# Value products spread over slots 15 to 20, and the last seven slots in a written order

## What is computed

```python
for t in range(S):
    y[:, :, t] = einsum('bhd,bhde->bhe', r_t, state + outer(u * k_t, v_t))
    state = w_t[:, :, :, None] * state + outer(k_t, v_t)
```

```python
h = gelu(x @ w_in)                       # 1024 wide
u, v = h[..., :512], h[..., 512:]
v_n = (v - mean(v)) / sqrt(var(v) + 1e-6) * g_ln
v_s = einsum('ts,bsd->btd', w_sg, v_n) + b_sg[None, :, None]
x = x + (u * v_s) @ w_out
```

## Time and profile before

| | |
|---|---|
| median of 3 runs | 373.62 us (372.19 to 373.78) |
| the profiled execution, its own time | 377.46 us |
| its span | 375.7 us |
| busy: PE, DVE, ACT, POOL | 95%, 63%, 48%, 20% |
| mean granted clock of PE | 0.973 |
| DMA | 23.73 MB, mean 63 GB/s |

### The profile page before, as it was taken

One profiled execution on the slowest core, in us unless ns is written; L12 is line 12 of the kernel. 1 busy time (PEld: TensorE's weight loads), 2 busy tenths in 40 slices (PEclk: granted clock), 3 DMA queues, 4 the chain that ended last, 5 costly groups with the idle time before them and its releaser, 6 DMA issues.

```text
span 375.7 us, 11261 instructions
## 1 busy us (share of the span) xinstructions
PE 358.4 (95%) x4909; PEld 332.9 (89%) x4909; DVE 236.2 (63%) x399; ACT 180.4 (48%) x310; POOL 74.5 (20%) x113
## 2 busy tenths in 40 slices
PE   8997987988799999999999999999999999999996
PEld 6766776877697788999899999999999999999996
DVE  5898778888773789675453679788953116752111
ACT  4754667776644366621240682378648003754000
POOL 6860210221000000000000026039600001951000
PEclk9999899999856999999999999999999999999999
DMA  8587852334210231300000040150000111000011
GB/s 249 161 214 225 248 145 63 85 59 89 56 35 0 36 96 24 75 2 0 0 2 0 2 167 3 29 202 2 0 2 0 44 42 42 2 0 2 21 58 48
DMA packets 39568, 23.73 MB, mean 63 GB/s; under 512 B 25568, under 2 KB 39008, under 8 KB 39520
## 3 DMA queue, kind: packets, MB, share of 16 engines
q1 hardware_dynamic: 39104, 23.02, 22.1%
q10 hardware_dynamic: 416, 0.00, 0.1%
HBM read 18.29 MB, written 2.36 MB: 55 GB/s over the span
## 4 chain that ended last, share of the span: by engine, by line
PE 93%; issue 4%; ACT 1%; DVE 0%; ACTq 0%
PE ps L1308 22%; PE ps L1309 22%; PE ps L1310 21%; PE ps L1298 11%; PE ps L1222 5%; PE ps L1245 3%; PE ps L1277 2%; PE ps L1256 2%; PE ps L1227 2%; PE ps L1232 1%; PE ps L1218 1%; PE ps L1269 1%; ACT yT L754 1%; ACT uT L780 0%; ACT wT L713 0%
## 5 line engine op out<-in xcount | busy, mean ns | idle before, releaser
L1298 PEld LDWEIGHTS ps<-r,kT 48*64 48x64 f32 x1920 | 35.5, 141 | 15.4 <-issue 13.5
L682 POOL TENSOR_TENSOR sq_f<-sq_f 128x384 f32<-128x384 f32 x32 | 33.8, 1072 | 74.9 <-ACT sq_f L824 74.8
L1298 PE MATMUL ps<-r,kT 48*64 48x32 f32 x1920 | 40.2, 226 | 6.8 <-issue 6.7
L1118 DVE TENSOR_TENSOR ot<-ps,ee 128x384 f32<-128x384 f32 x12 | 6.7, 558 | 54.6 <-PE ps L1310 54.6
L951 DVE TENSOR_TENSOR kT<-kT,wb 112x384 f32<-112x384 f32 x40 | 22.5, 564 | 19.1 <-PE ps L1298 18.6
L1103 DVE TENSOR_TENSOR sq_l<-sq_f,sq_h 128x384 fp32r<-128x384 f32 x32 | 27.6, 864 | 10.4 <-ACT sq_h L829 10.4
L1310 PE MATMUL ps<-xk_h,wk_l 128*128 128x384 f32 x96 | 32.2, 335 | 0.0
L1309 PE MATMUL ps<-xk_l,wk_h 128*128 128x384 f32 x96 | 32.2, 335 | 0.0
L1308 PE MATMUL ps<-xk_h,wk_h 128*128 128x384 f32 x96 | 32.2, 335 | 0.0
L1308 PE MATMUL ps<-wv_h,sq_h 128*128 128x384 f32 x96 | 32.1, 334 | 0.0
L1310 PE MATMUL ps<-wv_h,sq_l 128*128 128x384 f32 x96 | 32.1, 334 | 0.0
(11 more groups left out here) (158 smaller groups left out, 899.3 us busy)
## 6 DMA issues: line engine op xcount, KB each, us to landing
vt<-in_v_dram SPq DMA_DIRECT2D x32, 72.0 KB, 2.8
sgn<-in_moe_w_sg_dram SPq DMA_DIRECT2D x18, 128.0 KB, 2.9
out_dram<-ot SPq DMA_DIRECT2D x12, 192.0 KB, 1.9
raw_w<-in_w_dram SPq DMA_DIRECT2D x7, 288.0 KB, 4.3
raw_k<-in_k_dram SPq DMA_DIRECT2D x7, 288.0 KB, 5.0
raw_r<-in_r_dram SPq DMA_DIRECT2D x7, 288.0 KB, 5.4
xT<-yT SPq DMA_DIRECT2D x24, 72.0 KB, 2.3
win_raw<-in_moe_w_in_dram SPq DMA_DIRECT2D x12, 128.0 KB, 4.3
```

Source lines behind the costliest of these rows:

```text
L682: nc.gpsimd.tensor_tensor(t, t, t, ALU.mult).then_inc(k_sq, 1)
L1298: ins = nc.tensor.matmul(to[CHUNK[g], (x * C + c) * cols:(x * C + c + 1) * cols], kU[lo:hi, s] if l == 0 else kT[q % 4][lo:hi, s], rU[lo:h ...
```

## The change

PE's and ACT's lists for slots 14 to 21 are written out in LAST and ACT_LAST. V products stand one in each slot from 15 to 20; U products stand two in slot 20 and six in slot 21. In slot 15 the sg turn stands ahead of level (6,3). In slots 18 to 21 kt, u, yl and y of pairs 6 and 7 stand ahead of more of the early products. The casts of x for batch 0 go one each into slots 12, 13 and 14 on ACT, each waiting only for the stored rows that it reads; the subtractions x_l all into slot 14 on DVE. Statistics are taken one by one in slots 16 to 19, the last two with the norm at the start of slot 20 (ahead of the chain of pair 7); apply_norm for all six at the start of slot 21. Low parts: win_l for U in slots 17 and 18, wsg_l four in slot 19 and two in slot 21 (behind apply_norm). x_l moves behind gtmp in memory, the sgn ring is turned by two, and the waits follow. The warm-up products of pair 7 go.

```diff
         elif slot % 2 == 0:
-            jobs = [("level", a - 2, 4), ("kt", a - 3)] + EARLY_FIRST.get(slot, [])
+            jobs = [("level", a - 2, 4), ("kt", a - 3)]
...
-            (2, 0): 1, (2, 1): 1, **{(q, 1): 2 for q in range(3, NP)}}
-    GATE = {7: [("sg", 0)], 9: [("sg", 1)], 11: [("sg", 2)], 13: [("sg", 3)], 14: [("sg", 4)], 15: [("sg", 5)]}
-    EARLY_FIRST = {18: [("V", 0, 4)], 20: [("U", 0, 3)]}
-    EARLY_DENSE = {16: [("V", 0, 0), ("V", 0, 1)], 17: [("V", 0, 2), ("V", 0, 3)], 18: [("V", 0, 5)],
-                   19: [("U", 0, 0), ("U", 0, 1), ("U", 0, 2)], 20: [("U", 0, 4), ("U", 0, 5)],
-                   21: [("U", 0, 6), ("U", 0, 7)]}
-    ACT_LAST = {18: [("kt", 6), ("wm", 6), ("V", 0, 4), ("sy", 6), ("V", 0, 5)],
-                19: [("root", 0), ("y", 6), ("U", 0, 0), ("vn", 0), ("U", 0, 1), ("vn", 1), ("U", 0, 2), ("vn", 2)],
-                20: [("kt", 7), ("wm", 7), ("vn", 3), ("U", 0, 3), ("vn", 4), ("sy", 7), ("U", 0, 4), ("vn", 5), ("U", 0, 5)],
-                21: [("y", 7), ("U", 0, 6), ("U", 0, 7), ("high", 21)]}
+            (2, 0): 1, (2, 1): 1, **{(q, 1): 2 for q in range(3, NP - 1)}}
+    LAST = {14: [("level", 5, 4), ("kt", 4), ("level", 6, 2), ("sg", 4), ("level", 7, 0), ("u", 4)],
+            15: [("level", 5, 5), ("sg", 5), ("level", 6, 3), ("yl", 4), ("level", 7, 1), ("V", 0, 0), ("y", 4)],
+            16: [("level", 6, 4), ("kt", 5), ("level", 7, 2), ("V", 0, 1), ("u", 5)],
+            17: [("level", 6, 5), ("level", 7, 3), ("V", 0, 2), ("yl", 5), ("y", 5)],
+            18: [("level", 7, 4), ("kt", 6), ("V", 0, 3), ("u", 6)],
+            19: [("level", 7, 5), ("yl", 6), ("V", 0, 4), ("y", 6)],
+            20: [("V", 0, 5), ("kt", 7), ("U", 0, 0), ("u", 7), ("U", 0, 1)],
+            21: [("yl", 7), ("U", 0, 2), ("y", 7)] + [("U", 0, n) for n in range(3, 2 * FT)]}
+    ACT_LAST = {14: [("kt", 4), ("wm", 4), ("sg", 4), ("high", 14), ("x", 2), ("sy", 4)],
+                15: [("sg", 5), ("high", 15), ("V", 0, 0), ("y", 4)],
...
+                20: [("V", 0, 5), ("kt", 7), ("wm", 7), ("root", 0), ("U", 0, 0), ("sy", 7), ("U", 0, 1)],
+                21: [("U", 0, 2), ("y", 7), ("vn", 0)]
+                    + [job for n in range(1, C) for job in (("U", 0, n + 2), ("vn", n))] + [("high", 21)]}
...
-    LOW_SLOTS = {("inv", 0): 9, ("inv", 1): 11, ("inv", 2): 13, ("inu", 0): 16, ("inu", 1): 17, ("inu", 2): 17,
-                 ("sg", 0): 18, ("sg", 1): 18, ("sg", 2): 19, ("sg", 3): 20, ("sg", 4): 20, ("sg", 5): 21,
+    LOW_SLOTS = {("inv", 0): 9, ("inv", 1): 11, ("inv", 2): 13, ("inu", 0): 17, ("inu", 1): 18, ("inu", 2): 18,
+                 ("sg", 0): 19, ("sg", 1): 19, ("sg", 2): 19, ("sg", 3): 19, ("sg", 4): 21, ("sg", 5): 21,
...
-                act.wait_ge(yt_stored, stored_at(PPB * (b + 1) - 1))
+                act.wait_ge(yt_stored, stored_at(PPB * b + min(((m + 1) * P - 1) // (2 * D), PPB - 1)))
...
-                    dve.wait_ge(turned, turn_at[("sg", C - 1)] + 1)
+                    dve.wait_ge(turned, turn_at[("sg", RING)] + 1)
...
                 if slot == 20:
-                    apply_norm(0, range(3, 5))
+                    norm_stats(0, range(4, C))
+                    norm(0)
+                if slot == 21:
+                    apply_norm(0, range(C))
...
-                        if slot == 16:
-                            low_x(0, {4: 1, 2: 2}[l])
+                        if slot == 14 and l:
+                            low_x(0, {4: 0, 2: 1}[l])
...
-                if slot == 15:
-                    low_x(0, 0)
-                if slot == 17:
-                    norm_stats(0, range(4))
-                if slot == 18:
-                    norm_stats(0, range(4, C))
-                    norm(0)
-                if slot == 19:
-                    apply_norm(0, range(3))
-                if slot == 20:
-                    apply_norm(0, range(5, C))
+                if slot == 14:
+                    low_x(0, 2)
+                if 16 <= slot < 20:
+                    norm_stats(0, range(slot - 16, slot - 15))
```

More of the change, by code:

```diff
@@ L57, in pe_jobs @@
             jobs = FILL[slot]
+        elif slot in LAST:
+            jobs = LAST[slot]
         elif slot % 2 == 0:
-            jobs = [("level", a - 2, 4), ("kt", a - 3)] + EARLY_FIRST.get(slot, [])
+            jobs = [("level", a - 2, 4), ("kt", a - 3)]
             jobs += [("level", a - 1, 2), ("w", a + 1)] + GATE.get(slot, [])
@@ L64, in pe_jobs @@
             jobs += GATE.get(slot, []) + [("y", a - 3)]
-        jobs = [job for job in jobs if 0 <= job[1] < NP]
-        return jobs + EARLY_DENSE.get(slot, [])
+        return [job for job in jobs if 0 <= job[1] < NP]
     def side_jobs(slot):
@@ L83, in act_jobs @@
         jobs = [job for job in jobs if job[0] == "high" or 0 <= job[1] < NP]
-        return jobs + EARLY_DENSE.get(slot, [])
+        return jobs + [("x", 0)] * (slot == 12) + [("x", 1)] * (slot == 13)
     FILL = {0: [("level", 0, 0), ("w", 1)],
@@ L98, in rwkv_gmlp_channel_mix_kernel @@
     WARM = {(0, 2): 2, (0, 3): 1, (0, 4): 1, (0, 5): 1, (1, 0): 1, (1, 1): 1, (1, 2): 1, (1, 3): 1,
-            (2, 0): 1, (2, 1): 1, **{(q, 1): 2 for q in range(3, NP)}}
-    GATE = {7: [("sg", 0)], 9: [("sg", 1)], 11: [("sg", 2)], 13: [("sg", 3)], 14: [("sg", 4)], 15: [("sg", 5)]}
-    EARLY_FIRST = {18: [("V", 0, 4)], 20: [("U", 0, 3)]}
-    EARLY_DENSE = {16: [("V", 0, 0), ("V", 0, 1)], 17: [("V", 0, 2), ("V", 0, 3)], 18: [("V", 0, 5)],
-                   19: [("U", 0, 0), ("U", 0, 1), ("U", 0, 2)], 20: [("U", 0, 4), ("U", 0, 5)],
-                   21: [("U", 0, 6), ("U", 0, 7)]}
-    ACT_LAST = {18: [("kt", 6), ("wm", 6), ("V", 0, 4), ("sy", 6), ("V", 0, 5)],
[3 rows of a table removed]
+            (2, 0): 1, (2, 1): 1, **{(q, 1): 2 for q in range(3, NP - 1)}}
+    GATE = {7: [("sg", 0)], 9: [("sg", 1)], 11: [("sg", 2)], 13: [("sg", 3)]}
+    LAST = {14: [("level", 5, 4), ("kt", 4), ("level", 6, 2), ("sg", 4), ("level", 7, 0), ("u", 4)],
[6 rows of a table added]
+            21: [("yl", 7), ("U", 0, 2), ("y", 7)] + [("U", 0, n) for n in range(3, 2 * FT)]}
+    ACT_LAST = {14: [("kt", 4), ("wm", 4), ("sg", 4), ("high", 14), ("x", 2), ("sy", 4)],
[7 rows of a table added]
+                    + [job for n in range(1, C) for job in (("U", 0, n + 2), ("vn", n))] + [("high", 21)]}
     FIRST_TURNS = [("k", 0), ("r", 0), ("w", 0)]
@@ L288, in rwkv_gmlp_channel_mix_kernel @@
         x_h = up("x_h", [P, MT, S], F32R)
-        x_l = up("x_l", [P, MT, S], F32R)
         bbc = up("bbc", [P, S], F32)
         gtmp = [up(f"gtmp{x}", [P, HF], F32) for x in range(2)]
+        x_l = up("x_l", [P, MT, S], F32R)
         assert low[0] == A_aT
@@ L540, in load_sg @@
                 for j in range(3):
-                    sp.dma_start(sgn[:, t % RING, j * 2 * P:(j + 1) * 2 * P],
+                    sp.dma_start(sgn[:, (t + 2) % RING, j * 2 * P:(j + 1) * 2 * P],
                                  w_sg[t * P:(t + 1) * P, j * 2 * P:(j + 1) * 2 * P]).then_inc(sg_in[t], 16)
@@ L588, in _ @@
                     load_last_of_mlp()
-            sp.wait_ge(turned, turn_at[("r", NP - 1)] + 1)
+            sp.wait_ge(turned, turn_at[("sg", C - 1)] + 1)
             sp.dma_start(bbc[:, :], b_sg.rearrange("(a s) -> a s", a=1).broadcast_to([P, S])).then_inc(bias_in, 16)
@@ L877, in _ @@
                         lay_rows(job[1], job[2])
+                    elif job[0] == "x":
+                        high_x(0, job[1])
                     elif job[0] == "root":
@@ L883, in _ @@
                         copy_turn(job)
-                if slot == 14:
-                    for m in range(MT):
-                        high_x(0, m)
             for m in range(MT):
@@ L1232, in turn_job @@
                         ins = nc.tensor.transpose(dst[:, j // 3, (j % 3) * P:(j % 3 + 1) * P],
-                                                  sgn[:, q % RING, j * P:(j + 1) * P], ident[:, :])
+                                                  sgn[:, (q + 2) % RING, j * P:(j + 1) * P], ident[:, :])
                 ins.then_inc(turned, 1)
@@ L1320, in group_job @@
                 elif g < EARLY:
-                    turn_free([job for job in TURNS if turn_banks(job) is turn][-1])
+                    turn_free(("sg", C - 1))
                 if g == EARLY:
```

## The result

The changed kernel takes 378.04 us (377.59 to 381.4, 4 runs) against 373.70 us (372.19 to 374.58, 4 runs): a ratio of 1.014, 95% interval 1.0073 to 1.0207. It is slower. In a later comparison the same pair gave 378.85 against 373.47, 1.0184 (1.0136 to 1.0233). Forecast were 372.4 us and a range of 368.5 to 379: the time lies inside the range, on the other side of no change; slower had been given a chance of 0.30.

A forecast was written before the change was run, and what follows sets the result against it. PE was taken to bound the kernel, with low clock the largest loss ahead of G. Span 375.7 - 3.5 + 2.3 = 374.5, profiled run 376.3, median 372.4 us; range 368.5 to 379.

The forecast's parts named there:

- The steps inside the change: Slots 14 to 21 priced slot by slot at full clock, putting G's start at 150.8 instead of 154.3 us.
- the sum: Slots 14 to 21: priced PE work plus holes of 6.8 us at an unbroken clock, G starting at 150.8.
- 0.8 of code hole: Slot 15, inside level (6,3): late instruction code leaves about 0.8 us of the former 1.46 us hole.
- 0.45 of wait for DVE: Slot 15, after yl and ahead of level (7,1): PE waits 0.45 us for DVE to take level (5,5).
- The assumption that I called decisive: Slots 14 and 15: the clock stays up, as sg turn separates the holes, the longer is halved, dense V follows.
- Rival B: Low clock survives among the spread V products from slot 15 or 16: 375.8, 385 or 397 us; chance 0.18.
- If the first V does: Case where the first V lifts the clock: work from 101.3 to 105.1 takes 3.4 us more, 375.8 us.
- The span becomes 375.7 - 3.5 + 2.3: Whole span: 3.5 us gained ahead of G, 2.3 us lost to the clock, giving 374.5 us.
- about 8.3 went to the clock and small waits: Kernel before, 97.48 to 154.32: of 56.8 us, about 8.3 was clock loss and small waits.
- the 2.3 for the clock: Clock falls at G's start behind the 3.6 us hole: loss between 0 and 4.5 us, taken as 2.3.
- Rival C: Ahead of G: unprofiled runs have shorter code holes, so less to win; 374 to 376 us, chance 0.14.
- rival D: Ahead of G: the spread changes nothing, as PE's work is the same; 373.6 us, chance 0.06.

The follow-up runs named there:

- a_again: The changed kernel unchanged, run again for more runs and a trace: 378.85 us, 1.0184 of the kernel before.
- a_tail: Changed kernel with low parts of w_sg pieces 4 and 5 moved to slot 20 and ACT's vn casts one place earlier in slot 21: 373.17 us, 0.9972.
- a_chain: Changed kernel with low parts of w_sg pieces 2 and 3 moved from slot 19 to slot 20, behind the chain of pair 7: 378.03 us, 1.0086.
- a_slot15: Changed kernel with the first V put ahead of level (7,1) in slot 15: 378.30 us, 1.0088 of the kernel before.
- a_fill: Changed kernel with 16 warm-up products of 512 columns on PE between the last U product and G: 376.71 us, 1.0129.
- a_sg: Changed kernel with only the low parts of w_sg pieces 4 and 5 moved to slot 20, ACT's order kept: 376.26 us, 1.0111.
- a_all: Changed kernel with w_sg pieces 2 to 5 in slot 20, ACT's vn casts two places earlier, V ahead of level (7,1): 371.81 us, 0.9961.
- a_best: a_all with V ahead of yl of pair 6 in slot 19 and U ahead of yl of pair 7 in slot 21: 372.50 us, 0.9916.
- b_look2: The kernel before, unchanged, one more run traced for where its low-clock stretches lie: 381.36 us.
- b_again: The kernel before, unchanged, run and traced again: 373.08 us, 0.9968 of the kernel before.

## Why the prediction was wrong

**The steps inside the change were right.** Forecast and measured in the profile after: hole ahead of yl of pair 6, 0.65 and 0.76; of pair 7, 1.3 and 1.31; ahead of G, 3.6 and 3.72, ended by the subtraction named; a low clock behind G's start, 1.8 and 1.7 us of cost. G was put at 150.8 without low clock ahead of it, 54.4 us behind u, and came at 153.2. The same stretch took 55.55 us in a_again, without low clock: 1.2 us more than the sum, mostly holes (7.65 us against 6.8), among them two waits of 0.23 for ACT's copy of y that the sum doesn't have.

**Slot 15 was half right.** I had 0.8 of code hole and 0.45 of wait for DVE. The code came in time (only 0.11 ahead of yl), so PE was early and waited 1.41 for the same take of level (5,5): the sum is 0.3 off. The assumption that I called decisive, a clock that stays up, failed in this trace:

```profile
102.50:103.00 0.50, 0.50 (x30) 0.89 0.00 0
103.00:103.50 0.50, 0.50 (x2) 0.50 0.00 0
106.00:106.50 0.50, 0.50 (x3) 0.70 0.00 0
```

That is PE's clock by half microseconds in the changed kernel: it fell at 102.9 and was back at 106.3, while the first V ran. It cost 1.7 us. Rival B had "If the first V does", with 3.4 us more; it did, at half that price. In a_again, a_tail, a_chain, a_slot15, a_fill, a_sg, a_all and a_best, all with a V in slot 15, no fall came in slots 15 and 16 at all; a_slot15's came in slot 14. That is one of nine traces with 3.4 us in slots 15 and 16, against two of four with 17. It may be the spreading, but nine and four traces of something that comes and goes don't show it. Nor is the hole shown as the trigger: the same 1.46 us stood ahead of the fall in the forecast's trace and in b_look2, and in b_again no fall came behind it.

**The step that failed is the base of the sum.** "The span becomes 375.7 - 3.5 + 2.3": the 3.5 gained rests on "about 8.3 went to the clock and small waits", and the prediction carried the difference to the median over unchanged. Of those 8.3 us, 5.3 are the low stretch (57.90 against 52.65 us from u to G), which most runs don't have, and the same sum over b_again's rows leaves 3.1 for the rest. So the step counted as gained a low stretch that the typical run doesn't have, and carried that gain over to a median that was free of it. With b_again as the base, the forecast's own 54.4 us from u to G is 1.7 slower than 52.65, and with the 2.3 for the clock 4.0 slower: 377.7 us, where 378.04 was measured. Rival C named this stretch as shorter in the other runs, and priced it at 1.7 us, a third of what the rows show; its heading, shorter code holes, was the wrong cause. The warning was in plain view: the profiled run lay 3.8 us above the median of three runs, and a low-clock stretch was the largest loss in it.

**What the change won and lost ahead of G, at the full clock.** From u to G, b_again's holes add up to 4.2 us: 1.46, 0.32 and 0.56 ended by nothing that the profile shows, 1.26 for the third x_l, and 0.63 in two waits for ACT. In a_again the first kind is down to 0.45 and the wait for x_l is gone; waits for DVE have come in their place, 0.94, 0.76 and 1.32, with 0.46 for ACT: 3.9 in all. As far as the spreading goes that is rival D's case. The tail's 3.72 come on top, and the warm-up products take 0.54 off: 2.9 us, and 55.55 - 52.65 is 2.9. With 1.3 behind G it is 4.2 us slower by these two traces, against 4.3 and 5.4 measured. a_tail takes back 4.9. So the tail is shown as the cause, and the spread V products by themselves moved the typical time by nothing that these runs can tell (a_tail 0.9972, b_again 0.9968).

What the prediction cited from the Trainium skill (TensorE: Matmul & The Clock Gate, "What's actually happening"), that activity releases the throttle, agrees in kind with a_fill, which kept PE active through the tail and its clock at 1.00. It doesn't explain the 17 us at 1.2 GHz in the kernel before, over work that the rows show as busy. "Mostly hidden", said of code supply in the Trainium skill (Runtime: NRT & Kernel Launch, "Instruction fetch mechanics"), fits some stretches (0.11 us in slot 15 of the changed kernel) and not others (1.46 again in slot 15 of b_again).

## What to carry to other kernels

Before a forecast builds on a loss in one trace, ask whether it is in every run: a profiled time well above the median is a warning, and a few more traces of the unchanged kernel price it. Compare traces from one piece of common work to the next, not from the start of the span: ahead of u alone the four traces of the kernel before differ by 3.9 us (96.42 to 100.29). When an order is rewritten, follow the last product's path through every engine to the first consumer of the next stage, and put work that nobody waits for yet (here two subtractions) into the idle time ahead of it. A hole on TensorE is paid twice where the clock falls behind it.

## What the runs showed of the hardware

A hole of 2.09 us ahead of G (a_sg) was followed by 3.4 us at 1.2 GHz, and so was one of 3.72 in each of four traces; 0.53 (a_tail) and 0.25 (a_fill) were not. Elsewhere the hole doesn't decide it: behind 1.46 us in slot 15 the clock fell in two traces of the kernel before and stayed up in a third. Once down in slots 15 and 16 of the kernel before, it took 17 us to come back, through work that the trace shows as busy. It took 3.4 in slot 15 of the changed kernel, with a V product there, and 3.4 in slot 14 of a_slot15, with none. What sets the length is open.

The 17 us at half the clock cost 5.3 to 5.8 us and not 8.5, as waits of PE that stand at the full clock were covered. One kernel's runs differed by 8 us (371.28 to 379.27 in 35 runs of one session), and their mean clock between 0.964 and 0.995.

Holes inside levels, ended by nothing that the profile shows, recurred every 126 products or a multiple of it, and differed in length from trace to trace, from 0.2 to 1.5 us; that they come from the supply of code is argued from that count and wasn't tested by a run. Not every hole marked "issue" is one of them: the 1.26 us ahead of V in b_again ends with DVE's third x_l.
